# The start of a three-layer kernel: weight splits, a root and its spread in another order, and the spatial weights split one stage later

## What is computed

```python
kv = einsum('bhsd,bhse->bhde', k, v)             # 8 batches, 8 heads, 576 rows, 64 columns
out = einsum('bhsd,bhde->bhse', q, kv)
x = out / sqrt(mean(out*out, -1) + 1e-6) * g_norm    # -> (8, 576, 512)

h = maximum(x @ w_in, 0); u, v = h[..., :512], h[..., 512:]
v_n = (v - mean(v)) / sqrt(var(v) + 1e-6)
x = (u * (einsum('ts,bsd->btd', w_spatial, v_n) + b_spatial[None, :, None])) @ w_out

h = maximum(x @ w_in2, 0)
y = (h * sigmoid(conv3(h, conv_w))) @ w_out2
```

## Time and profile before

| | us |
|---|---|
| median of 3 runs | 831.85 |
| lowest, highest | 831.42, 832.64 |
| the profiled execution, its own time | 832.46 |
| its span in the trace | 830.7 |
| PE busy | 811.2 |
| mean granted clock of PE, as a share of full | 0.992 |

### The profile page before, as it was taken

The page is one execution under the profiler, slowest core; times in us unless marked ns, Lnnn a source line. Parts: engine busy times, 40 slices in busy tenths (PEclk is TensorE's granted clock), DMA queues, the critical chain, the costliest instruction groups (busy, mean ns, idle before and its releaser), DMA issues.

```text
span 830.7 us, 15568 instructions
## 1 busy us (share of the span) xinstructions
PE 811.2 (98%) x6102; PEld 731.3 (88%) x6102; DVE 467.2 (56%) x945; ACT 386.5 (47%) x674; POOL 39.0 (5%) x44
## 2 busy tenths in 40 slices
PE   8699999999999999999999999999999999999998
PEld 7468979898897979899999898998989899898996
DVE  3758565555746655666449275282834819166370
ACT  3436353433526253442537374372834637265461
POOL 3413000000000000000050000000000000000000
PEclk9789999999999999999999999999999999999999
DMA  9742352434244352314030111203012030120001
GB/s 318 277 136 109 101 187 73 165 104 159 72 119 165 86 199 72 144 42 130 1 115 2 54 55 39 83 1 108 2 38 82 0 107 0 51 70 19 32 0 63
DMA packets 24661, 74.29 MB, mean 89 GB/s; under 512 B 2386, under 2 KB 2610, under 8 KB 20660
## 3 DMA queue, kind: packets, MB, share of 16 engines
q1 hardware_dynamic: 24484, 73.84, 26.9%
q10 hardware_dynamic: 144, 0.01, 0.0%
HBM read 54.84 MB, written 19.00 MB: 89 GB/s over the span
## 4 chain that ended last, share of the span: by engine, by line
PE 91%; DVE 5%; DMA 1%; ACT 1%; issue 1%; SPq 0%; ACTq 0%
PE ps L385 49%; PE ps L545 24%; PE ps L416 11%; PE ps L336 3%; PE ps L352 2%; DMA kv_raw<-kv_rest_dram 1%; PE ps L486 1%; PE ps L364 1%; DVE bn_stats L898 1%; DVE r L862 0%; DVE work L918 0%; DVE v_hg_split L924 0%; DVE vrs L916 0%; PE ps L474 0%; DVE r L870 0%
## 5 line engine op out<-in xcount | busy, mean ns | idle before, releaser
L385 PE MATMUL ps<-x_gated_split,w_product_split 128*128 128x288 f32 x1536 | 204.8, 295 | 0.0
L385 PEld LDWEIGHTS ps<-x_gated_split,w_product_split 128*128 128x128 f32 x1536 | 204.3, 188 | 0.5
L545 PE MATMUL ps<-w_in_split,v_hg_split 128*128 128x512 f32 x832 | 194.7, 390 | 0.0
L545 PEld LDWEIGHTS ps<-w_in_split,v_hg_split 128*128 128x128 f32 x832 | 155.8, 188 | 31.9
L1027 DVE SCALAR_TENSOR_TENSOR work<-work,const_cols 128x576 f32<-128x576 f32 x64 | 52.4, 819 | 151.3 <-ACT work L778 151.3
L385 PE MATMUL ps<-w_sp_split,v_hg_split 128*128 128x288 f32 x896 | 120.2, 295 | 1.3 <-DVE w_sp_split L947 1.3
L385 PEld LDWEIGHTS ps<-w_sp_split,v_hg_split 128*128 128x128 f32 x896 | 119.2, 188 | 1.5 <-issue 1.5
L385 PE MATMUL ps<-x_gated_split,w_in_split 128*128 128x288 f32 x768 | 104.4, 296 | 1.3 <-ACT work L636 1.3
L385 PEld LDWEIGHTS ps<-x_gated_split,w_in_split 128*128 128x128 f32 x768 | 102.2, 188 | 3.4 <-ACT work L636 1.7
L416 PE MATMUL ps<-w_in_split,x_gated_split 128*128 128x512 f32 x384 | 93.4, 397 | 0.0
L416 PEld LDWEIGHTS ps<-w_in_split,x_gated_split 128*128 128x128 f32 x384 | 70.5, 188 | 20.4 <-issue 6.1
(11 more groups left out here) (96 smaller groups left out, 699.1 us busy)
## 6 DMA issues: line engine op xcount, KB each, us to landing
kv_raw<-kv_main_dram SPq DMA_DIRECT2D x8, 2048.0 KB, 8.8
q_raw<-q_T_dram SPq DMA_DIRECT2D x8, 1152.0 KB, 5.1
gated_scratch<-work SPq DMA_DIRECT2D x32, 288.0 KB, 2.1
q_raw<-gated_scratch SPq DMA_DIRECT2D x8, 1152.0 KB, 5.6
out_dram<-o_x SPq DMA_DIRECT2D x32, 256.0 KB, 2.0
sq_then_r<-r_scratch SPq DMA_DIRECT2D x14, 576.0 KB, 6.2
kv_raw<-kv_rest_dram SPq DMA_DIRECT2D x8, 256.0 KB, 8.9
work<-w_in_dram SPq DMA_DIRECT2D x2, 1024.0 KB, 14.3
```

The costliest lines, as they stand in the source:

```text
L385: last = pe.matmul(pair[bank][:, c, :], st, mo[:, c * HALF:(c + 1) * HALF], start=(n == 0), stop=(n == len(steps) - 1))
L545: last = pe.matmul(PS[:, ROW_BANK[i], :], x, wout2[:, w, f, :], start=(f == 0 and n == 0), stop=(f == FT - 1 and n == len(PASSES) - 1))
```

## The change

Nothing is added to or taken from the arithmetic. What moves:

- ACT's `W_hi(0)`, `W_hi(1)` and DVE's `W_lo(0)`, `W_lo(1)` go ahead of batch 0's o copies and squares.
- All four `w21_hi` stand ahead of `root(0)` on ACT, and `w21_lo(1)` ahead of `mean_square(0)` on DVE. ACT then waits for the finished root (s_r) ahead of `win_hi(0)`, and `win_hi(2)`, `win_hi(3)` stand behind the first two `x_hi`.
- `spread_r` is run in pairs (0, 1), then (2, 3); the two of a pair write two halves of the banks, and only the second pair waits for `x_scale`. `w_product(2)` stands between the pairs and `w_product(3)` behind the second. DVE scales two pairs at a time.
- In batch 0's body, the five `sp_hi` leave the v stage. Two now stand behind `u_relu(0)` and three behind `v_hi` of v's last tile, ahead of `b_hi`. POOL's list is the same, but each of its subtractions waits for its `sp_hi`.

```diff
             def spread_r(m):
                 if m == 0:
                     pe.wait_ge(s_selT, 4)
                     pe.wait_ge(s_r, 1)
-                else:
-                    pe.wait_ge(s_xm, m)
+                if m == 2:
+                    pe.wait_ge(s_xm, 2)
...
-                        last = pe.matmul(PS[c * D:(c + 1) * D, R_BANK + g, 0:QS], selT[r, m, :], r0[r, c, :], start=True, stop=True)
+                        last = pe.matmul(PS[c * D:(c + 1) * D, R_BANK + g, (m % 2) * QS:(m % 2 + 1) * QS], selT[r, m, :], r0[r, c, :],
+                                         start=True, stop=True)
...
-            for m in range(MT):
-                spread_r(m)
-                if m < 2:
-                    w_product(2 + m)
+            spread_r(0)
+            spread_r(1)
+            w_product(2)
+            spread_r(2)
+            spread_r(3)
+            w_product(3)
...
-                    if first:
-                        sp_hi(i)
                 u_relu(b, 0)
+                if first:
+                    sp_hi(0)
+                    sp_hi(1)
                 u_relu(b, 1)
                 v_hi(b, NT - 1)
                 if first:
+                    for j in (2, 3, 4):
+                        sp_hi(j)
                     b_hi()
...
             kv_copy(0)
+            W_hi(0)
+            W_hi(1)
             for m in range(MT):
                 o_copy(0, m)
-            w21_hi(0)
-            w21_hi(1)
+            for j in range(MT):
+                w21_hi(j)
             root(0)
-            w21_hi(2)
-            w21_hi(3)
-            for n in range(4):
-                W_hi(n)
-            for j in range(MT):
-                win_hi(j)
+            W_hi(2)
+            W_hi(3)
+            act.wait_ge(s_r, 1)
+            win_hi(0)
+            win_hi(1)
+            x_hi(0, 0)
+            x_hi(0, 1)
+            win_hi(2)
+            win_hi(3)
             W_hi(4)
-            x_hi(0, 0)
             W_hi(5)
-            x_hi(0, 1)
-            W_hi(6)
             x_hi(0, 2)
             x_hi(0, 3)
+            W_hi(6)
             W_hi(7)
...
-                    dve.wait_ge(s_rP, m + 1)
+                    dve.wait_ge(s_rP, (m // 2 + 1) * 2)
```

More of the change, by code:

```diff
@@ L873, in x_scale @@
                 if isinstance(a, int) and a == 0:
-                    dve.wait_ge(s_rP, m + 1)
+                    dve.wait_ge(s_rP, (m // 2 + 1) * 2)
                     o_q = o_T[:, m, :].rearrange("p (g t) -> p g t", g=4)
-                    dve.scalar_tensor_tensor(out=o_q, in0=o_q, scalar=g_col, in1=PS[:, R_BANK:R_BANK + 4, 0:QS],
+                    dve.scalar_tensor_tensor(out=o_q, in0=o_q, scalar=g_col, in1=PS[:, R_BANK:R_BANK + 4, (m % 2) * QS:(m % 2 + 1) * QS],
                                              op0=ALU.mult, op1=ALU.mult).then_inc(s_xm, 1)
@@ L992, in _ @@
             kv_copy(0)
+            W_lo(0)
+            W_lo(1)
             for m in range(MT):
@@ L995, in _ @@
             w21_lo(0)
+            w21_lo(1)
             mean_square(0)
-            w21_lo(1)
             w21_lo(2)
             w21_lo(3)
-            W_lo(0)
             inverse_root(0)
-            for n in (1, 2, 3):
-                W_lo(n)
+            W_lo(2)
             dve.wait_ge(s_const_in, DMA)
             x_scale(0, 0)
+            x_scale(0, 1)
+            W_lo(3)
+            x_lo(0, 0)
+            x_lo(0, 1)
+            x_scale(0, 2)
+            x_scale(0, 3)
             W_lo(4)
-            x_scale(0, 1)
-            x_lo(0, 0)
             W_lo(5)
-            x_scale(0, 2)
-            x_lo(0, 1)
-            x_scale(0, 3)
-            W_lo(6)
             x_lo(0, 2)
             x_lo(0, 3)
+            W_lo(6)
             W_lo(7)
```

## The result

| | before | changed |
|---|---|---|
| median, 6 runs each on one chip | 831.95 us | 825.06 us |
| lowest, highest | 828.35, 832.75 | 824.44, 825.14 |
| profiled execution | 832.46 | 825.10 |
| its span | 830.7 | 823.3 |

The ratio is 0.9915, with a 95% interval of 0.9898 to 0.9931: faster by 6.9 us, 0.85%.

What follows compares the result with a forecast made beforehand. PE was taken to bound the kernel, its early waits costing their length plus slow clock. Terms: -12.9 us at v, +2.7 spatial wait, +1.8 clock, together -8.4, so 831.85 became 823.4 us; range 820.6 to 827.0.

Steps and rivals of the forecast that it cites:

- w_product(0) and (1) without a wait, at full clock: Prologue on PE: both products run from 27.14 to 33.2 without idling, 3.01 us each.
- inverse_root at the short end, 3.8 us: Batch 0's root on DVE: 3.8 us instead of 7.06, since POOL's work waits behind it; r0 at 32.65.
- Spreads, POOL's w_in, kv_product: Prologue: first two spreads end at 34.1, POOL's half of w_in at 39.9, kv_product starts at 41.0.
- Head of the v stage at 43.7: Batch 0's v stage starts at 43.7 instead of 56.60, a gain of 12.9 us; range 43.6 to 44.6.
- the 16.8: Time from the start of batch 0's v stage to its u stage, taken from the kernel before: 16.8 us.
- The wait ahead of spatial: Between batch 0's u and spatial stages: PE waits 5.0 us instead of 1.30; spatial starts 18.0 us after u's start.
- The 2.7: Term of the sum: 2.7 us lost to the spatial wait, 5.0 against 1.30 + 0.74, and rounding.
- The clock behind the wait: Spatial stage of batch 0: a slow clock behind the wait costs 1.8 us; range 0.8 to 2.6.
- My three cases: Prologue products of the kernel before, behind waits: 5.25, 4.60 and 4.08 us against 3.01, 3.01 and 2.55, costing 1.5 to 2.2.
- rival 1: U stage: POOL doesn't block the root, so spatial starts 1.7 us earlier; 821.2 us; chance 0.13.
- Rival 2: Prologue: the clock falls there too, and two products cost 2.2 and 1.6 us more; 827.2 us; chance 0.14.
- Rivals 3 and 4: 3: root or POOL's w_in bounds prologue, 828 to 829 us, chance 0.07; 4: low clock stays, 840 us, chance 0.03.

Runs made afterwards that it cites:

- e5: Changed kernel without ACT's wait for the finished root ahead of win_hi(0); 824.69 us.
- e1: Changed kernel with only the spatial part undone: the five sp_hi stand in batch 0's v stage again; 819.83 us.
- e2: Kernel before the change with only the spatial part of the change made; 836.83 us.
- e4: Changed kernel with sp_hi(0) and sp_hi(1) moved from the u stage back into the v stage, the other three left; 823.80 us.
- e3: Changed kernel with 18 added matmuls whose result nobody reads, on PE between batch 0's u stage and the wait for the spatial weights; 822.91 us.
- e6: Changed kernel with W's tiles 0 and 1 read out where the kernel before did it, around the root; 827.00 us.
- e9: Changed kernel with the spreads one at a time again, and W_lo(3) ahead of the second scaling; 828.45 us.
- e10: Changed kernel with six added matmuls whose result nobody reads, on PE in the 1.75 us wait ahead of batch 0's square_sum; 825.14 us.
- e7: e1 with the bias row's two steps also in the v stage: b_hi behind sp_hi(1), its subtraction behind tile 2's normalisation; 821.63 us.

## Why the prediction was right, point by point

- **w_product(0) and (1) without a wait, at full clock**: right. From the end of square_sum the two were put at 6.0 us and took 5.73. The early W_hi and W_lo fitted in: o_copy started at 20.80, and the squares without a delay.
- **inverse_root at the short end, 3.8 us**: right (3.76), and it was the right choice between 3.8 and 7.06. The reason was half right: in e5, without ACT's wait for the root, it took 4.8 us and not 7.06, with one step blocked, and the time stayed the same. The wait gives the last 1.0 us of the root, and nothing of the kernel's time.
- **Spreads, POOL's w_in, kv_product**: right in order; two spreads end at 33.3 (34.1 in the sum), POOL's half of w_in is done at 39.4 (39.9), kv_product starts at 39.77 (41.0 was the sum; square_sum ended 0.2 earlier, and groups of matmuls overlap by more than I had allowed for).
- **Head of the v stage at 43.7**: it started at 42.78, but the tile then waited 0.78 for DVE's copy of k^T v. I had the x_lo under POOL's block as a bound (up to 44.6), and missed that the copy stands behind W_lo(6) and W_lo(7) in DVE's list, and behind a split that the sum doesn't have at all, that of x's last rows. It took 0.42 us before the change and 1.50 now, beside POOL's subtraction of the first half of w_in (L310, from 42.09):

```profile
42.65 1.50 DVE L897 TENSOR_TENSOR rest_split<-o_x,rest_split 128x256 fp32r<-128x256 f32 x1
```

The u stage, which counts, came at 60.66, where 60.5 was forecast. That is closer than the working deserved: v was 0.9 us early and its first tile 1.1 us longer than the 16.8 had it, and the two errors cancelled.
- **The wait ahead of spatial**: right in mechanism and size. 18.0 us from u's start was forecast, 18.17 measured; 5.0 of waiting, 5.20 measured; the two blocked steps of the root and the last three subtractions of POOL are in the trace, and e1 and e2 show that the wait comes from this half of the change alone. e4 shows that the first two subtractions block another step when they are moved into the v stage, so that the gain there is 0.4 us and not 1.7. One working in the sum doesn't come out: 5.0 less 1.30 and 0.74 is 2.96. The 2.7 that was used follows from the starts of the spatial stage, 12.9 less 10.2, and is the right one.
- **The clock behind the wait**: the mechanism was right (e3), the size was off: 1.8 forecast, 17.62 - 15.08 = 2.54 measured, near the end of my bounds. I had sized it by waits of 2 to 3.5 us in the prologue, but the length of the wait doesn't settle the price: behind the same 5.2 us the 112 matmuls took 16.58 us in e6, 16.96 in e9, 17.35 in e10, 17.83 in e2 and 17.89 in e5, which is 1.5 to 2.8 us above 15.08. My three cases came from a single execution, too. e2 has the same prologue, and there the second product took 3.03 us after a wait of 2.14, and kv_product 2.55 after the same two short waits. With 0.16 at u and 0.17 in the spatial stage's start, this 0.74 is the whole of the 1.0 us by which the profiled execution missed (825.10 against 824.1).
- **Rivals**: rival 1 (no block) fell by the trace. Rival 2 (clock falls in the prologue) is real in a third of the traces of the experiments, but doesn't cost the 3.8 us that I gave it: the products lose 7.34 - 5.73 = 1.6, and the first v tile, which then waits for nothing, gives all of it back by the start of u. Rivals 3 and 4 didn't come.

## What to carry to other kernels

A wait of TensorE is priced at its length and at the clock behind it, and the second part varies: 2.54 us behind 5.20, 2.15 behind 2.40 (e6), nothing behind 2.14 (e2); a step that is moved off one path needs a place where its own engine and each engine it can block are free, or the gain comes back as a wait elsewhere (e4, e7). When several edits come together, make each alone: here a gain of some 12 us hid a loss of 4 to 5, and taking the loss back and fitting the moved steps in gave 9 us more. When a wait is removed upstream, look at what the next consumer has queued in front of it (W_lo(6), W_lo(7) ahead of the copy), since it is that which is late next.

## What the runs showed of the hardware

- Matmuls that nobody needs can pay for themselves: 18 of them in a 5.2 us wait took 2.15 us off the kernel, since the stage behind ran at full clock.
- The same list of matmuls had its clock fall in some executions and not in others, after a wait of 1.75 us and 64 short matmuls; it cost the two products 1.6 us. The kernel before shows a spread of its own, 828.35 to 832.75, and e2's trace, with the same prologue as the kernel before, had its second w_product at 3.03 us instead of 4.60. Why an execution falls on one side isn't settled by these runs.
- Behind a wait of the same 5.2 us the same 112 matmuls took 16.58 to 17.89 us in six traces, against 15.01 to 15.12 at full clock.
- A subtraction on a single partition took 1.99 us instead of 0.76 beside a subtraction of POOL's, and a step with one input (L868) 1.28 instead of 0.31.
